# Three reads of the expert table at the top of TensorE's loop over pairs, in place of two at each pair

## The reference

```python
def _moe_ref(x, w_gate, w1, w2) -> np.ndarray:
    ...
    logits = x @ w_gate
    expert_idx = np.argmax(logits, axis=1)
    ...
    for e in range(E):
        mask = expert_idx == e
        ...
        xe = x[mask]
        h = np.maximum(xe @ w1[e], 0.0)
        ye = h @ w2[e]
        out[mask] = gate_w[mask, None] * ye
```

## Time and profile before

| | |
|---|---|
| median of 3 runs | 807.64 us (804.0 to 810.27) |
| the profiled execution | 808.7 us |
| its span | 807.0 us |
| TensorE busy with matmuls | 744.9 us, 92% |
| granted TensorE clock, mean | 0.976 |
| loops over pairs (3 to 28) | 244 to 442 us of the span |

### The profile page before, as it was taken

How to read it: one execution, slowest core, us unless ns; L and a number is a source line. 1 busy time by engine, 2 the same in 40 slices (tenths; PEclk the granted TensorE clock), 3 DMA queues, 4 the chain that set the end, 5 groups by cost and what they waited for, 6 DMA issues and landing times.

```text
span 807.0 us, 17962 instructions
## 1 busy us (share of the span) xinstructions
PE 744.9 (92%) x6435; PEld 551.7 (68%) x6436; DVE 518.1 (64%) x1346; ACT 415.4 (51%) x811; POOL 192.6 (24%) x286
## 2 busy tenths in 40 slices
PE   4899999995488999999999899999999999999994
PEld 3688888885277888888888655556566555565552
DVE  6769898897887457565687565465465455554441
ACT  4578777767753458455664233343433433434332
POOL 4477787874221101111100000020100100100101
PEclk9999999998699999999999999999999999999998
DMA  6879979660527965887220000000000000000000
GB/s 195 221 232 294 326 234 340 184 203 26 176 69 266 358 219 198 262 317 256 84 83 1 2 2 1 0 34 1 25 9 2 32 0 0 32 0 0 34 1 32
DMA packets 39517, 95.87 MB, mean 119 GB/s; under 512 B 7150, under 2 KB 19630, under 8 KB 39438
## 3 DMA queue, kind: packets, MB, share of 16 engines
q1 hardware_dynamic: 31010, 66.33, 26.3%
q10 hardware_dynamic: 5788, 19.47, 6.7%
q0 software_dynamic: 2640, 9.01, 3.4%
HBM read 70.92 MB, written 23.89 MB: 117 GB/s over the span
## 4 chain that ended last, share of the span: by engine, by line
PE 83%; DVE 7%; DMA 3%; issue 3%; ACT 2%; SPq 1%; POOL 1%; ACTq 0%; DVEq 0%; POOLq 0%
PE bank L1694 34%; PE bank L1836 19%; PE bank L1728 12%; PE bank L1557 4%; PE bank L1581 4%; PE bank L1603 1%; PE bank L1684 1%; PE bank L1567 1%; PE bank L1573 1%; DMA slot<-qkT 1%; PE bank L1547 1%; DMA d_x<-og 1%; PE bank L1549 1%; PE bank L1813 1%; ACT slot L787 1%
## 5 line engine op out<-in xcount | busy, mean ns | idle before, releaser
L1694 PE MATMUL bank<-stage,slot 128*128 128x512 f16 x768 | 181.1, 379 | 0.0
L1836 PE MATMUL bank<-slot,dec 128*128 128x320 f16 x768 | 159.1, 299 | 0.0
L1694 PEld LDWEIGHTS bank<-stage,slot 128*128 128x128 f16 x768 | 75.1, 98 | 74.3 <-DVE stage L1489 0.2
L1694 PE MATMUL bank<-qbd,slot 128*128 128x128 f16 x1984 | 117.9, 221 | 7.4 <-issue 6.9
L1694 PEld LDWEIGHTS bank<-qbd,slot 128*128 128x128 f16 x1984 | 113.7, 99 | 11.0 <-issue 10.5
L1493 DVE TENSOR_TENSOR qk<-stage,dec 128x512 f16<-128x512 f32 x96 | 66.4, 692 | 84.7 <-ACT dec L989 84.7
L1836 PE MATMUL bank<-slot,qk 128*128 128x320 f16 x384 | 114.8, 299 | 0.0
L703 POOL DMA_INDIRECT out<-stage,tok_i x24 | 23.6, 983 | 368.6 <-ACT stage L1000 364.7
L989 ACT CAST dec<-stage 128x512 f16<-128x512 f32 x96 | 59.4, 619 | 100.7 <-PE bank L1836 72.0
L1489 DVE TENSOR_TENSOR stage<-bank,stage 128x512 f32<-128x512 f32 x96 | 66.2, 690 | 67.4 <-ACT stage L983 66.9
L983 ACT ACTIVATE stage<-bank 128x512 f32<-128x512 f32 x96 | 57.3, 597 | 97.5 <-PE bank L1694 96.5
(11 more groups left out here) (268 smaller groups left out, 1192.1 us busy)
## 6 DMA issues: line engine op xcount, KB each, us to landing
slot<-d_w SPq DMA_DIRECT2D x12, 1280.0 KB, 6.4
stage<-wB SPq DMA_DIRECT2D x6, 1280.0 KB, 8.3
d_w<-slot ACTq DMA_DIRECT2D x6, 1280.0 KB, 8.3
stage<-wA SPq DMA_DIRECT2D x6, 1024.0 KB, 6.5
d_w<-slot SPq DMA_DIRECT2D x4, 1280.0 KB, 8.7
stage<-wB ACTq DMA_DIRECT2D x4, 1280.0 KB, 9.3
qk<-qkT SPq DMA_DIRECT2D x12, 360.0 KB, 5.7
slot<-qkT SPq DMA_DIRECT2D x12, 360.0 KB, 8.0
```

What stands on the lines that cost most here:

```text
L1694: ins = t_.matmul(pf, a[:, col:col + P], x(k), start=(q == 0), stop=(q == len(ops) - 1))
L1836: ins = t_.matmul(bank[4 + q][:, 0:DM], x[f % 2][:, q * P:(q + 1) * P], slotB[2 + f // NF][:, c0:c0 + DM], start=(f == 0 and z == 0), stop ...
```

## The change

`pair` no longer reads the table; it is given both numbers, of its own pair (`now`) and of the pair before (`before`). In a loop's turn the three numbers of the pairs p - 1, p and p + 1 are read at the top and kept in registers. Before, the top pair read p and p - 1 and the middle pair p + 1 and p, four reads a turn. Pairs outside of the loops read two as before, at the same place.

```diff
                 n = (hi - lo) // 2 * 2
                 if n:
                     with pe.Fori(lo, lo + n, 2) as p:
+                        e = [expert(p + i) for i in range(-1, 2)]
                         for i in range(2):
-                            pair(p + i, (lo + i) % 2)
+                            pair(p + i, (lo + i) % 2, e[i + 1], e[i])
                 if lo + n < hi:
-                    pair(hi - 1, (hi - 1) % 2)
-
-            def pair(p, i, unit=None):
-                now, before = expert(p), expert(p - 1)
+                    pair(hi - 1, (hi - 1) % 2, expert(hi - 1), expert(hi - 2))
+
+            def pair(p, i, now, before, unit=None):
                 h_product(p, i, now)
                 if unit is not None:
                     sums(unit)
```

More of the change, by code:

```diff
@@ L1789, in _ @@
             x_turn(3, 1)
-            pair(2, 0)
+            pair(2, 0, expert(2), expert(1))
             at = 3
@@ L1793, in _ @@
                 pairs(at, p)
-                pair(p, p % 2, PAIR_SCALE[p])
+                pair(p, p % 2, expert(p), expert(p - 1), PAIR_SCALE[p])
                 at = p + 1
```

## The result

The changed kernel takes 813.33 us (median of 14 runs, 811.13 to 816.83), the kernel before 808.27 us (14 runs, 804.0 to 811.53). The ratio is 1.0065 with a 95% interval of 1.0047 to 1.0084, about +5.3 us. The profiled execution took 813.06 us, with a span of 811.3 us.

The account below looks back on a forecast made before the run. In the loops the array and, for 5.7 us, the sequencer feeding it were taken to set the end. Terms 7.7 - 0.3 + 0.3 - 0.8 = +6.9 us on 807.64 gave 814.5 us, +0.85%; range 808.5 to 818.5.

Parts of the forecast that it names:

- a change of the stalls in pairs 12 to 14: Stalls there are of the size of the effect; their changing would make the whole prediction wrong.
- The added read: At each of 11 loop tops, one more read lies bare: 0.7 us net each, 7.7 us in all.
- a long read at pair 3: At top pair 3 the third read may be long too, costing 0.6 us or nothing: +0.3 us taken.
- spare at three tops: Tops 10, 14 and 23, first turns of their loops, have 0.1 us each to spare: -0.3 us.
- The removed reads: At 10 of 11 middle pairs worth nothing, being hidden; at pair 6 two long reads go: -0.8 us.
- 5.7 us of idle time: Array idle time between 244 and 442 us put down to the sequencer: 5.1 ahead of first products, 0.6 ahead of second.
- rival B: Time saved in middle pairs carries over to the next top: +0.2 to -2.6 us, 805 to 808; chance 0.05.
- Rival A: Longer idle time at pair 3 makes the clock fall there, slower by over 1%: +8.8 us, 816.4; chance 0.33.
- Rival C: Pair 13's stall, taken for late instructions, goes with its lower clock as code shifts: +3.2 us, 810.8; chance 0.11.

Follow-up runs that it names:

- e3: Changed kernel with a fourth, unused read at each loop top, none in the middle pair; ratio 1.024 against the kernel before.
- e1: Kernel before with two reads at the loop top as before, but only one in the middle pair; ratio 0.9962 against the kernel before.
- e2: Changed kernel with three reads at the top and one read put back in the middle pair; ratio 1.0077 against the kernel before.
- e8: Changed kernel with 5 more matmuls in the wait ahead of pair 0, moving all code behind; ratio 1.0104 against the kernel before.
- e11: Changed kernel with 8 more matmuls in the wait ahead of pair 0, moving all code behind; ratio 1.0119 against the kernel before.
- e9: e5 with 8 more matmuls in the wait ahead of pair 0, moving all code behind; ratio 0.9939 against the kernel before.
- e5: Kernel before with each number read once, by its own pair, and kept in a register for the next; ratio 1.0006 against the kernel before.
- e4: Kernel before with no top reads; middle pair reads two numbers, kept in registers over the branch back; ratio 0.9979 against the kernel before.
- e7: Kernel before with 8 more matmuls in the wait ahead of pair 0, moving all code behind; ratio 1.0026 against the kernel before.

## Why the prediction was right

**The forecast** of +6.9 us stands against +5.3 us measured; 814.5 against 813.33 us. Sign, size and place were right. The mechanism was the one that was forecast, a bare read at each top. How near the total came is in part luck: it rests on what pair 13 did in this kernel, and the prediction had named a change of the stalls in pairs 12 to 14 as what would make it wrong.

**The added read** was put at 0.7 us net, 7.7 us over the tops; +0.3 us for a long read at pair 3 and -0.3 us for spare at three tops cancel. The trace shows 7.7: 0.54 and 0.55 us at the tops with spare (0.15 each, 0.1 taken), 0.66 to 0.72 at the seven others, 1.27 at pair 3, where 1.0 was expected. There the third read took 545 ns and the first two 1089 and 933; the sequencer was ready for the product 0.9 us later than before (246.9 and 247.8 us), and the array came to the transposes 0.37 us earlier. e3 shows the same price again (8.1 us for one more at each top), and e1 that without it there is no loss.

**The removed reads** were put at nothing but 0.8 us at pair 6. It was 0.75 us. e2, with one of them put back, is slower by less than the intervals can tell, and not by the 7 us that the read in each middle pair would cost if it were bare. Of the 5.7 us of idle time that the prediction counts to the loops, 2.4 us belong to pair 13, which is outside of them; no term of the sum rests on that.

**No carrying over** (rival B): shown by the distances of e1 and by the changed kernel itself. Its line 1680, which stands behind the handing over of the second product, comes at 414.2 us (behind middle pair 24's first product), 422.2 us (behind top pair 25's) and 429.4 us (behind middle pair 26's), each 1.0 to 1.2 us after the start of the second product; the rows are

```profile
L1680 PEldq ALU_OP  x2: 36/36/36, 414.2 to 422.2; - x2
L1703 PEldq FUSED_REGOPS  x2: 37/37/37, 417.5 to 422.8; - x2
...
L1680 PEldq ALU_OP  x1: 36/36/36, 429.4 to 429.4; - x1
```

At the middle pair the sequencer is ready for the first product at 422.8, 1.9 us before the array takes it at 424.75, while at the top it is ready at 417.5, just ahead of the array's 417.58. Of this lead of 1.9 us nothing is left at 429.4 us.

**Rival A** met its condition and not its effect in the profiled execution. Pair 3 idled for 2.57 us, more than the 2.14 us behind which the clock fell before, and the 64 matmuls behind it ran at full pace. In e2 (2.60 us idle) and e8 (3.08 us) the clock did fall there; in e11 (3.02 us) and e3 (3.25 us) it did not. Over the runs the mean granted clock is no lower with the change (0.978 over 14 runs; before 0.977 to 0.978 over 11 to 23), since pair 13's fall went at the same time. Behind pair 13's stalls it is the same: a fall after 1.97 us in e1, none after 2.32 us in e9. So the length of the idle time doesn't decide it, and what does is open. The price was right: e8's 64 matmuls take 5.37 us there in place of 3.74.

**Rival C** is what the sum missed, as a part of the outcome and not in place of it. It was given 3.7 us for a stall that goes, with its lower clock; 2.7 us came back in pair 13, because the stall moved and shrank (1.0 us) and the clock did not fall behind it (1.6 us). The experiments show that the stalls belong to a place in the code, and that moving the code can cost or give back time. How much of the changed kernel's total is owed to it they show less well: the same change measures 0.65% at the place where it was made and 0.9% with all code 8 matmuls further on, and these differ by less than their intervals; e8, which put pair 13's stall back 5 matmuls into the product, did not bring the 2.7 us back. The mean of the three kernels with three reads at the top and the loops' code at other places (e2, e8, e11) is 1.010 of before. The transfer itself takes about 1 us, and the array goes on 2.2 to 2.5 us after it starts. Open is why it starts late at some places and not at most others. Traffic may play a part, as pair 13's stretch has a DMA share near 1, but it isn't needed throughout: the last 1.5 us of the stall in e5's pair 11 (304.0 to 305.5) have a mean share of 0.05.

## What to carry to other kernels

A register read in a hardware loop costs nothing where the sequencer has a lead over the array and its whole 0.7 us where that lead is used up, which is first of all at the loop's top, where the branch back stands too. Fewer reads a turn can therefore be slower; put them one at each place with cover, or keep a number in a register over the branch, which took the loss off the tops in e4, e5 and e9. Below 1%, compare a version at two or three places of its code before believing it: moving all code by 8 matmuls changed three kernels here by +0.3, +0.5 and -0.7%.

## What the runs showed of the hardware

- A read of one number of a table in SBUF by TensorE's sequencer takes 296 to 318 ns in the load in most cases (median 306 in the kernel before), and 0.65 to 0.8 us with its address, folding and check instructions. Some loads take 0.5 to 1.1 us, in the kernel before at 244 to 246, 268 to 271 and 319 to 321 us on TensorE and VectorE alike, where the DMA share is 0.8 or more.
- A head start of 1.9 us over the array is lost within a product of 64 matmuls of 128 columns.
- Code that runs for the first time can hold up the array at fixed places of the program, in the middle of matmuls (0.2 to 3.4 us; 2.14 in the kernel before, 3.43 in e5) or in a branch of the sequencer (2.56 us, e7). In the eleven stalls of pair 13, in e5's pair 11 and behind e7's branch, a transfer of instructions of 0.02 MB starts 2.2 to 2.5 us before the array goes on. The two places in e5 are three times 256 instructions and 3 apart. Later turns of a loop didn't show such a stall inside a product, and with the loops written out the kernel was 1.7% slower.
- The clock fell from its upper to its lower level behind idle times of the array of 1.97 us (e1), 2.14 us (before), 2.60 us (e2) and 3.08 us (e8), and stayed up behind 2.32 us (e9), 2.57 us (changed), 3.02 us (e11) and 3.25 us (e3).
